# A reciprocal of the reverse decay scans in place of the forward decay scans, in a three-block forward pass on one Trainium2 core

## The reference

```python
# block 1: decayed linear attention, 8 heads of 48 columns
for t in range(S):
    state = alpha[:, :, t, :, None] * state + einsum('bhd,bhe->bhde', k[:, :, t], v[:, :, t])
    y[:, :, t] = einsum('bhd,bhde->bhe', q[:, :, t], state)
# block 2: a gated MLP with a mixing over the sequence
h = gelu(x @ w_in); u, v = split(h)
v_s = einsum('ts,bsd->btd', w_sg, layernorm(v) * g_ln) + b_sg
x = x + (u * v_s) @ w_out
# block 3: the real part of a 2D FFT, then a normalised MLP
u = x + real(fft2(x)); out = u + relu(layernorm(u) @ w_ch1) @ w_ch2
```

## Time and profile before

| | us |
|---|---|
| median of three executions | 788.97 |
| lowest and highest | 788.46, 790.69 |
| the profiled execution, device time | 788.8 |
| its span in the trace | 787.0 |
| TensorE busy in the span | 746.0 |
| VectorE busy in the span | 465.9 |
| ScalarE busy in the span | 194.6 |
| GpSimd busy in the span | 75.3 |

### The profile page before, as it was taken

One profiled execution on the slowest core, in us unless ns is written; L12 is line 12 of the kernel. 1 busy time (PEld: TensorE's weight loads), 2 busy tenths in 40 slices (PEclk: granted clock), 3 DMA queues, 4 the chain that ended last, 5 costly groups with the idle time before them and its releaser, 6 DMA issues.

```text
span 787.0 us, 12141 instructions
## 1 busy us (share of the span) xinstructions
PE 746.0 (95%) x4900; PEld 723.0 (92%) x4900; DVE 465.9 (59%) x1015; ACT 194.6 (25%) x366; POOL 75.3 (10%) x123
## 2 busy tenths in 40 slices
PE   4779999999999999999996699999999999999997
PEld 4668899989999899999996699999999999999997
DVE  5787877689675978747656763537263534432121
ACT  1212521133111331124223242123212232112111
POOL 1011100011000210014004112000210010000000
PEclk9889999999999999999999799999999999999999
DMA  7432322321312231215228021201220010000000
GB/s 228 142 95 79 98 80 55 111 76 46 91 46 76 76 91 47 76 64 161 81 74 268 11 61 36 66 1 34 78 82 1 30 60 0 30 4 27 1 31 31
DMA packets 20986, 54.02 MB, mean 69 GB/s; under 512 B 2484, under 2 KB 14792, under 8 KB 20936
## 3 DMA queue, kind: packets, MB, share of 16 engines
q1 hardware_dynamic: 17416, 42.52, 17.8%
q0 software_dynamic: 2816, 9.10, 3.8%
q10 hardware_dynamic: 704, 1.71, 0.7%
HBM read 43.86 MB, written 9.46 MB: 68 GB/s over the span
## 4 chain that ended last, share of the span: by engine, by line
PE 87%; DVE 6%; DMA 4%; issue 1%; ACT 1%; POOL 0%; DVEq 0%; SPq 0%
PE bank L1039 73%; PE bank L1090 4%; DMA decay_k_q<-in_akq 3%; PE bank L1065 3%; PE bank L1086 2%; PE bank L1078 2%; PE bank L1221 1%; PE bank L1055 1%; PE bank L1111 1%; DVE u_kept L1000 1%; PE bank L1045 1%; DMA u_new<-x_scratch,mirrored_rows 1%; DVE fwd L795 1%; DVE rev L781 1%; DVE w_in_lo L767 0%
## 5 line engine op out<-in xcount | busy, mean ns | idle before, releaser
L1039 PE MATMUL bank<-ut_hi,w_c_parts 128*128 128x384 f32 x576 | 163.9, 340 | 1.3 <-DVE ut_lo L977 1.3
L991 DVE SCALAR_TENSOR_TENSOR hidden_lo<-bank,hidden_hi 128x384 fp32r<-128x384 f32 x96 | 53.3, 555 | 126.5 <-ACT hidden_hi L714 125.4
L1039 PEld LDWEIGHTS bank<-ut_hi,w_c_parts 128*128 128x128 f32 x576 | 105.6, 188 | 1.5 <-issue 1.5
L1039 PE MATMUL bank<-w_c_hi,hidden_hi 128*128 128x384 f32 x288 | 97.1, 337 | 0.7 <-DVE u_kept L1000 0.7
L1039 PE MATMUL bank<-w_c_lo,hidden_hi 128*128 128x384 f32 x288 | 96.7, 336 | 0.0
L1039 PE MATMUL bank<-w_c_hi,hidden_lo 128*128 128x384 f32 x288 | 96.7, 336 | 0.0
L1039 PE MATMUL bank<-ut_lo,w_c_parts 128*128 128x384 f32 x288 | 96.5, 335 | 0.0
L714 ACT ACTIVATE hidden_hi<-bank 128x384 fp32r<-128x384 f32 x96 | 47.3, 492 | 199.2 <-PE bank L1039 199.2
L1039 PE MATMUL bank<-w_sg_hi,vn_hi 128*128 128x384 f32 x192 | 66.1, 344 | 0.7 <-ACT u_gelu L647 0.7
L1039 PE MATMUL bank<-w_sg_hi,vn_lo 128*128 128x384 f32 x192 | 64.2, 335 | 0.0
L1039 PE MATMUL bank<-w_sg_lo,vn_hi 128*128 128x384 f32 x192 | 64.2, 334 | 0.0
(11 more groups left out here) (167 smaller groups left out, 1493.8 us busy)
## 6 DMA issues: line engine op xcount, KB each, us to landing
decay_k_q<-in_akq SPq DMA_DIRECT2D x21, 672.0 KB, 5.2
x_scratch<-x_half SPq DMA_DIRECT2D x8, 579.0 KB, 3.6
out_tiles<-u_kept SPq DMA_DIRECT2D x24, 192.0 KB, 2.0
values<-in_v SPq DMA_DIRECT2D x18, 192.0 KB, 5.2
x_quarters<-x_scratch SPq DMA_DIRECT2D x16, 168.9 KB
raw_weights_b<-in_w_second SPq DMA_DIRECT2D x3, 768.0 KB, 4.2
u_new<-x_scratch SPq DMA_DIRECT2D x4, 576.0 KB
decay_k_q_b<-in_akq SPq DMA_DIRECT2D x3, 672.0 KB, 8.4
```

The costliest lines, as they stand in the source:

```text
L991: nc.vector.scalar_tensor_tensor(out=hid[1][:, i % 4, :], in0=HB[i % 2][:, 0:HS], scalar=0.0, in1=f32(hid[0][:, i % 4, :]), op0=ALU.max, o ...
L1039: ins = nc.tensor.matmul(dst, a, c, start=start and n == 0, stop=stop and n == len(passes) - 1)
```

## The change

The four forward scans of a chunk, the reciprocal of `g_end` from which they start and the two waits between them are taken out. One reciprocal of all 512 columns of `rev` takes their place; its result `inv` lies in the buffer in which `fwd` lay, and `qu` reads it. The wait for `g_end` moves from prep to carry, the only step that still reads it. The semaphores and the small tile g_inv go. The change is on VectorE alone: each of the 24 chunks has 4 instructions fewer there.

```diff
-            for name, shape in (("fwd", [PR, G, P]), ("rev", [PR, G, P]), ...
+            for name, shape in (("inv", [PR, G, P]), ("rev", [PR, G, P]), ...
...
                     nc.vector.tensor_tensor(kd[:], raw[:, 1], rev[:], ALU.mult).then_inc(kd_done, 1)
+                    nc.vector.reciprocal(inv[:], rev[:]).then_inc(inv_done, 1)
+                if step == "query":
+                    dve.wait_ge(inv_done, i + 1)
+                    need(dve, y_done, before)
+                    nc.vector.tensor_tensor(qu[:], raw[:, 2], inv[:], ALU.mult).then_inc(qk_done, 1)
+                if step == "carry":
+                    m = (NT - 1) * n + c
                     dve.wait_ge(g_end_done, i + 1)
-                    nc.vector.reciprocal(g_inv[:], g_end[:, c % 2]).then_inc(g_inv_done, 1)
-                    dve.wait_ge(g_inv_done, i + 1)
-
-                    for g in range(G):
-                        ins = nc.vector.tensor_tensor_scan(fwd[:, g, :], raw[:, 0, g, :], zeros[:],
-                                                           g_inv[:, g:g + 1], ALU.mult, ALU.add)
-                    ins.then_inc(fwd_done, 1)
-                if step == "query":
-                    dve.wait_ge(fwd_done, i + 1)
-                    need(dve, y_done, before)
-                    nc.vector.tensor_tensor(qu[:], raw[:, 2], fwd[:], ALU.mult).then_inc(qk_done, 1)
-                if step == "carry":
-
-                    m = (NT - 1) * n + c
```

More of the change, by code:

```diff
@@ L174, in build @@
         g_blk = place("g_end_by_block", [PR, G, 2], F32, region(32))
-        g_inv = place("g_inv", [PR, G], F32, region(16))
         blk = place("head_of_row", [PR, 2], F32, region(8))
@@ L202, in attention_set @@
             bufs = {"raw": place("decay_k_q" + tag, [PR, 3, G, P], F32, at_raw)}
-            for name, shape in (("fwd", [PR, G, P]), ("rev", [PR, G, P]), ("kd", [PR, G, P]), ("qu", [PR, G, P]),
+            for name, shape in (("inv", [PR, G, P]), ("rev", [PR, G, P]), ("kd", [PR, G, P]), ("qu", [PR, G, P]),
                                 ("kn", [P, G, PR]), ("sm", [P, G, 2, P])):
@@ L290, in build @@
         g_end_done = sem("g_end_done")
-        g_inv_done = sem("g_inv_done")
-        fwd_done = sem("fwd_done")
+        inv_done = sem("inv_done")
         g_blk_done = sem("g_blk_done")
@@ L771, in attend @@
                 i = NT * n + c
-                raw, fwd, rev, kd, qu, sm = (bufs[x] for x in ("raw", "fwd", "rev", "kd", "qu", "sm"))
+                raw, inv, rev, kd, qu, sm = (bufs[x] for x in ("raw", "inv", "rev", "kd", "qu", "sm"))
                 before = i if inputs is None else i - 1
@@ L789, in attend @@
                     nc.vector.tensor_tensor(kd[:], raw[:, 1], rev[:], ALU.mult).then_inc(kd_done, 1)
-                    dve.wait_ge(g_end_done, i + 1)
-                    nc.vector.reciprocal(g_inv[:], g_end[:, c % 2]).then_inc(g_inv_done, 1)
-                    dve.wait_ge(g_inv_done, i + 1)
-                    for g in range(G):
-                        ins = nc.vector.tensor_tensor_scan(fwd[:, g, :], raw[:, 0, g, :], zeros[:],
-                                                           g_inv[:, g:g + 1], ALU.mult, ALU.add)
-                    ins.then_inc(fwd_done, 1)
+                    nc.vector.reciprocal(inv[:], rev[:]).then_inc(inv_done, 1)
                 if step == "query":
-                    dve.wait_ge(fwd_done, i + 1)
+                    dve.wait_ge(inv_done, i + 1)
                     need(dve, y_done, before)
-                    nc.vector.tensor_tensor(qu[:], raw[:, 2], fwd[:], ALU.mult).then_inc(qk_done, 1)
+                    nc.vector.tensor_tensor(qu[:], raw[:, 2], inv[:], ALU.mult).then_inc(qk_done, 1)
                 if step == "carry":
                     m = (NT - 1) * n + c
+                    dve.wait_ge(g_end_done, i + 1)
                     nc.vector.tensor_tensor(g_blk[:], g_end[:, c % 2].unsqueeze(2).to_broadcast([PR, G, 2]),
```

## The result

| | before | with the reciprocal |
|---|---|---|
| median, us | 789.57 (4 runs) | 805.31 (4 runs) |
| lowest and highest, us | 788.46, 790.69 | 803.49, 808.23 |
| the profiled execution, device time, us | 788.8 | 804.15 |
| its span, us | 787.0 | 802.3 |

The ratio is 1.0215, with a 95% interval of 1.0194 to 1.0235: the change costs 15.7 us by the medians and 15.3 us by the two spans of the profiled executions. The forecast was 804 us.

A forecast was written before the change was run, and what follows sets the result against it. TensorE, busy 95% of the span, was taken to bound the steady part, VectorE and loads the start. Terms of 5.4 + 2.8 + 7.2 = 15.4 us on 788.8 us gave 804 us, range 792 to 828 us.

The forecast's parts named there:

- The price of the reciprocal: On VectorE, 512 columns at six passes, 6.3 ns each: 3.37 us, so each chunk's prep grows by d = 1.55 us.
- The rivals of one pass: Pipelined division on VectorE: the reciprocal costs what kd costs, 0.68 us, kernel 784 us; one or two passes had chance 0.12.
- of eight: Eight passes a column on VectorE: reciprocal 4.44 us, kernel 819 us, or 826 us with a fifth chunk's stall; chance 0.20.
- The start: The first 47.6 us, where the wait chain runs through VectorE and loads: 3.5 times d of 1.55 us, 5.4 us lost.
- Between 0 and d I count half: In the start, the third chunk's load, issued d = 1.55 us later, was taken to land half of d later.
- Beside batch 0: Chunks prepared beside block 2: second chunk loses 1.3 us after 0.28 us of room, third the whole 1.55; together 2.8 us.
- The 17 chunks: Number of the 24 chunks said to be prepared beside block 2 from 90 to 330 us, with one 0.8 us wait.
- Beside batches 1 and 2: Delays add up through the single raw buffer; TensorE is 3.6 us late by the fourth chunk, twice: 7.2 us.
- the loads leave no room from there on: Beside batch 2, the third chunk's load lands as the next rev starts, so the fourth chunk starts 4.65 us late.
- I stop there: the next chunk has more room: Beside batches 1 and 2, no loss was counted after the fourth chunk, where TensorE is 3.6 us late.
- The sum: Start 5.4, batch 0 2.8, batches 1 and 2 7.2: 15.4 us on 788.8 us, giving 804 us.
- The signs I named: VectorE busy about 500 us or more, qu waits about 8 us, first products about 53 us, fourth rev waiting beside batch 2.

The follow-up runs named there:

- recip_start: The kernel before with the reciprocal only in the six chunks of batch 0, the 18 others keeping their scans: 791.37 us, ratio 1.0042.
- early_load: The changed kernel with the 18 loads beside block 2 split, alpha and k leaving once kd is done, q after qu: 801.22 us, ratio 1.0157.
- late_recip: The changed kernel with the reciprocal moved from the prep step to the query step, just ahead of qu: 810.14 us, ratio 1.0272.

## Why the prediction was right

**The price of the reciprocal.** Forecast 3.37 us from the surplus of a 4-column one at six passes a column, measured 3.35 us. A price of about six passes a column is right; the working was luckier than it looks. The fit of the 4-column row said 5.7 ns, which gives 3.07 us; the choice of 6.3 ns was a rounding up. From 128 to 512 columns the slope is 6.35 ns, and the short instruction, from which I had worked, lies off that line. The rivals of one pass (0.68 us) and of eight (4.44 us) are out. On the Trainium skill: "VectorE: DVE Perf Modes", section "First, the fixed hardware budget", gives Reciprocal a repeat count of 8. The trace agrees that a column is repeated work, 6.35 ns against 1.05 ns for `kd`, but, read as passes, it makes about six of it, not eight, and the measurement decides. The Trainium skill's page "Vector Engine (DVE) Microarchitecture Reference", section 3.2, lets the chain span all eight slices; my reading of it as one column a clock is contradicted by the same row.

**The start.** Forecast 5.4 us, 4.4 us in the profile. By the chain the three reciprocals behind the third chunk's load give 3 x 1.53 = 4.6 us, that load lands 0.5 us earlier, and the fifth chunk's load takes 0.5 us longer (6.90 instead of 6.38 us). The term "Between 0 and d I count half" failed: the load left 1.53 us later and landed 0.5 us earlier. Over 13 traces it lands at the same time within 0.9 us wherever it leaves between 11.45 and 13.23 us, so the term should have been nothing. In recip_start it lands at 22.06 us and the first product stands 5.1 us late.

**Beside batch 0.** Forecast 1.3 + 1.55 us. TensorE waits 1.27 us at the second chunk, and 2.27 us at the third, 1.5 us more than the 0.8 us of before. Right in both. (The 17 chunks that I counted from 90 to 330 us are 16 by the starts of `rev`; nothing rests on it.)

**Beside batches 1 and 2.** Forecast 2 x 3.6 us; the profile has 5.5 us (1.1 + 179.42 to 278.51 us against 171.00 to 264.54, less the next first chunk's 1.1) and 4.7 us. I had put 2.1 us at the second chunk, nothing at the third and 1.5 us more at the fourth. TensorE waits 1.1 and 0.9 us for `qu` of the first and second chunk, 2.1 us together as forecast though not all at the second, and nothing at the third. At the fourth the size is about as forecast, the wait another: from the third scores to the fourth it takes 2.0 us longer beside batch 1 and 1.3 us longer beside batch 2, but TensorE has stopped for gated_lo, ahead of the scores, and then finds `qu` ready.

```profile
221.41 0.45 PE L1032 MATMUL bank<-w_out_hi,gated_hi 128*128 128x384 f32 x1 [1.75 <-DVE gated_lo L836]
...
251.81 0.41 PE L1032 MATMUL bank<-w_out_hi,gated_hi 128*128 128x384 f32 x1 [0.98 <-DVE x_half L844]
```

```profile
312.05 1.36 DVE L779 TENSOR_TENSOR_SCAN rev<-decay_k_q,zeros 112x127 f32<-112x127 f32 x4 [1.93 <-DMA decay_k_q<-in_akq]
...
319.70 0.44 PE L1032 MATMUL bank<-w_out_hi,gated_hi 128*128 128x384 f32 x1 [0.94 <-DVE gated_lo L836]
```

That the loads leave no room from there on was right, and early_load shows it. Wrong was "I stop there: the next chunk has more room": steps behind `qu` have less room. Behind the fifth chunk's scores TensorE stops again, for x_half (0.98 and 0.7 us), and from there to the sixth's it takes 1.2 and 1.0 us longer. That is most of the 3 us by which these stretches came out dearer than forecast.

**The sum.** The terms came out as 4.4 + 2.9 + 5.5 + 4.7 = 17.5 us up to the last scores, 2 us above the 15.4 us: 1.0 us less in the start, 3.0 us more beside batches 1 and 2. The total agreed because the rest of the program was 2.2 us shorter in this execution than in the one before. The path that I named is the one that was lost on, but that the total came within 1 us of the forecast is luck.

**The signs I named.** VectorE's busy time rose to 501.3 us, `rev` of the fourth chunk beside batch 2 waits 1.93 us for its load, the waits for `qu` rose to 7.6 us ("about 8 us"; my own terms add up to 10.8 us, and the 4.4 us for gated_lo and x_half stand for the rest), and the first product starts at 52.06 us ("about 53 us").

## What to carry to other kernels

Fewer instructions are not less time: one reciprocal of 512 columns costs nearly twice the four scans and the small reciprocal that it replaces, and a short instance of an operation in the trace already tells roughly, if its surplus over a plain operation of that width is divided by its columns (here 5.7 ns, against 6.35 ns measured). An engine at 59% beside one at 95% has room only instruction by instruction; where a buffer's reload waits for the last reader, a delay there can come back in the next round, so follow the loop of reader, load and next use, and count all steps behind it, not only the one that the change touches. Where work can be moved, put the long part where its engine idles, not right ahead of the one who waits.

## What the runs showed of the hardware that I had not expected

- A load that was issued 1.53 us later landed 0.5 us earlier (10.76 us became 8.70 us); over 13 traces it lands at 21.4 to 22.3 us whether it leaves at 11.5 or at 13.1 us. The same load issued at 9.79 us, ahead of two weight loads, took 5.5 us.
- The reciprocal's price is not linear in its width: 170 ns at 4 columns, 908 ns at 128, 3346 ns at 512. Cut in four it occupies VectorE as long as whole (27.08 - 23.78 = 3.30 us against 3.27).
- After a wait of 2.3 us TensorE ran nine to ten products at the lower of its clock levels in one kernel and not in another with the same wait, 1.6 us for it. In late_recip, behind a wait of 2.0 us, nine products took 3.99 us at that level and 2.16 us at the other.
